# The last output tile taken as three tiles of 128 steps

## The reference

```python
def _moe2_ref(x, w_in, g_ln, w_sg, b_sg, w_out):
    h = gelu_tanh(x @ w_in)                      # (2, 768, 1024)
    u, v = h[..., :512], h[..., 512:]
    v_n = (v - mean(v)) / sqrt(var(v) + 1e-6) * g_ln
    v_s = einsum('ts,bsd->btd', w_sg, v_n) + b_sg[None, :, None]
    gated = u * v_s                              # (2, 768, 512)
    return x + gated @ w_out                     # (2, 768, 384)
```

## Time and profile before

| | before |
|---|---|
| median of 3 executions | 333.68 us (333.19 to 333.71) |
| the profiled execution's own time | 332.61 us |
| its span, first to last instruction | 330.9 us |
| PE busy | 320.0 us, 97% |
| DVE busy | 197.2 us, 60% |
| ACT, POOL busy | 151.0 us, 46%; 98.1 us, 30% |
| mean granted TensorE clock | 0.999 of full speed |
| output transfers L502 | 12 of 192 KB, median 1.9 us from issue to landing |

### The profile page before, as it was taken

The page is one execution under the profiler, slowest core; times in us unless marked ns, Lnnn a source line. Parts: engine busy times, 40 slices in busy tenths (PEclk is TensorE's granted clock), DMA queues, the critical chain, the costliest instruction groups (busy, mean ns, idle before and its releaser), DMA issues.

```text
span 330.9 us, 6786 instructions
## 1 busy us (share of the span) xinstructions
PE 320.0 (97%) x2684; PEld 299.5 (91%) x2684; DVE 197.2 (60%) x331; ACT 151.0 (46%) x301; POOL 98.1 (30%) x94
## 2 busy tenths in 40 slices
PE   6987899999999999999999999999999999999996
PEld 2657889999999999999999998899999988999996
DVE  4869999983696398639416055991643546123432
ACT  5446844553845455465547592755113025311100
POOL 5530344004314211430032050672233018313220
PEclk9999999999999999999999999999999999999999
DMA  7979033232304401300006036000000210000012
GB/s 230 408 259 350 27 124 125 87 130 61 144 2 165 166 5 24 144 9 2 6 9 240 0 110 246 29 0 0 2 0 0 97 49 0 2 0 2 0 48 95
DMA packets 11153, 28.09 MB, mean 85 GB/s; under 512 B 1232, under 2 KB 5872, under 8 KB 9840
## 3 DMA queue, kind: packets, MB, share of 16 engines
q1 hardware_dynamic: 10976, 27.51, 23.7%
q10 hardware_dynamic: 144, 0.14, 0.1%
HBM read 24.74 MB, written 2.36 MB: 82 GB/s over the span
## 4 chain that ended last, share of the span: by engine, by line
PE 84%; DVE 7%; ACT 3%; issue 2%; DMA 2%; POOL 0%; SPq 0%; ACTq 0%; DVEq 0%
PE pm L297 16%; PE pm L298 15%; PE pm L299 15%; PE ps L613 3%; PE ps L297 3%; PE ps L299 3%; PE ps L298 3%; PE py L691 3%; PE pkt L638 3%; PE py L677 2%; PE pkt L297 2%; PE pkt L299 2%; PE pu L297 2%; PE pu L299 2%; PE pkt L298 2%
## 5 line engine op out<-in xcount | busy, mean ns | idle before, releaser
L542 POOL TENSOR_TENSOR k_l<-sq,k_h 128x512 fp32r<-128x512 f32 x24 | 31.9, 1332 | 79.2 <-ACT sq L944 79.2
L297 PE MATMUL pm<-xkr_h,wk_h 128*128 128x256 f32 x144 | 42.1, 292 | 0.0
L297 PE MATMUL pm<-k_h,wv_h 128*128 128x256 f32 x144 | 41.2, 286 | 0.4 <-POOL k_l L542 0.4
L299 PE MATMUL pm<-k_h,wv_l 128*128 128x256 f32 x144 | 40.7, 283 | 0.0
L298 PE MATMUL pm<-k_l,wv_h 128*128 128x256 f32 x144 | 40.7, 283 | 0.0
L298 PE MATMUL pm<-xkr_l,wk_h 128*128 128x256 f32 x144 | 40.7, 283 | 0.0
L299 PE MATMUL pm<-xkr_h,wk_l 128*128 128x256 f32 x144 | 40.7, 282 | 0.0
L533 POOL TENSOR_TENSOR rkp<-inw 128x512 f32<-128x512 f32 x12 | 15.3, 1281 | 62.7 <-DVE r_in L1132 62.7
L936 ACT ACTIVATE relu<-pm 128x512 f32<-128x512 f32 x24 | 14.3, 596 | 36.2 <-PE pm L299 36.1
L595 POOL TENSOR_TENSOR gated_l<-gf,gated_h 128x384 fp32r<-128x384 f32 x16 | 16.4, 1025 | 46.1 <-ACT gated_h L1055 36.1
L1187 DVE SCALAR_TENSOR_TENSOR xf<-X,omu,xf 128x256 f32<-128x256 f32 x36 | 19.5, 554 | 15.4 <-ACT xf L902 15.4
(11 more groups left out here) (239 smaller groups left out, 880.4 us busy)
## 6 DMA issues: line engine op xcount, KB each, us to landing
inw<-in_units SPq DMA_DIRECT2D x10, 1026.5 KB, 5.0
vb<-in_vT SPq DMA_DIRECT2D x12, 256.0 KB, 5.0
wsg_raw<-in_wsgT SPq DMA_DIRECT2D x1, 2304.0 KB, 8.8
out_y<-y_out SPq DMA_DIRECT2D x12, 192.0 KB, 1.9
wk_raw<-in_moe_w_k SPq DMA_DIRECT2D x3, 512.0 KB, 9.9
wv_raw<-in_moe_w_v SPq DMA_DIRECT2D x4, 384.0 KB, 7.0
win_raw<-in_moe_w_in SPq DMA_DIRECT2D x3, 512.0 KB, 4.6
inw<-in_units SPq DMA_DIRECT2D x2, 512.0 KB, 5.5
```

The lines of the kernel that those rows point to most:

```text
L297: pe.matmul(o, a_h, b_h, start=first and n == 0, stop=False, skip_group_check=True)
L299: mm = pe.matmul(o, a_l, b_h, start=False, stop=last and n == len(pairs) - 1, skip_group_check=True)
L542: pool.tensor_tensor(k2_l[:, 2 * n:2 * n + 2], sq[:, j % 2].rearrange("p (g t) -> p g t", g=2), k2_h[:, 2 * n:2 * n + 2], ALU.subtract).th ...
```

## The change

The last entry of the list, ("o", 1, 2, 1), is replaced by three entries ("e", 1, 2, 0), ("e", 1, 2, 1) and ("e", 1, 2, 2). Each covers the same 128 channels and 128 of the 384 steps, and takes the next bank of the ring (7, 0 and 1), one addition of 128 x 128 into the next `y_out` buffer and one transfer of 64 KB. All other tiles keep their order, banks and sizes. The function `out_steps` gives the range of steps of a tile of either kind.

```diff
--- before.py
+++ after.py
@@ -352,6 +352,12 @@
                     ORDER2 += [(x, b, f, h) for h in range(HALVES) for f in range(GT)]
                 if x == "o":
                     ORDER2 += [("o", b, t, h) for h in range(HALVES) for t in range(KT)]
+
+        ORDER2[-1:] = [("e", B - 1, KT - 1, n) for n in range(HALF // C)]
+
+        def out_steps(kind, y):
+
+            return slice(HALF + y * C, HALF + (y + 1) * C) if kind == "e" else slice(y * HALF, (y + 1) * HALF)
         TILES2 = [t for t in ORDER2 if t[0] != "x"]
 
         def filled2(eng, *tile):
@@ -497,10 +503,11 @@
             load_part(sp, len(WSPLIT) - 1)
             n = 0
             for kind, b, x, y in TILES2:
-                if kind == "o":
+                if kind in "oe":
                     emptied2(sp, kind, b, x, y)
-                    sp.dma_start(outT[x * P:(x + 1) * P, b * S + y * HALF:b * S + (y + 1) * HALF],
-                                 y_out[:, n % 3, :]).then_inc(s_out[n % 3], 16)
+                    at = out_steps(kind, y)
+                    sp.dma_start(outT[x * P:(x + 1) * P, b * S + at.start:b * S + at.stop],
+                                 y_out[:, n % 3, 0:at.stop - at.start]).then_inc(s_out[n % 3], 16)
                     n += 1
             for j in range(3):
                 sp.wait_ge(s_out[j], 16 * len(range(j, n, 3)))
@@ -843,8 +850,10 @@
                     if x == 0:
                         pe.wait_ge(gh_done, GT * HALVES * b + GT * (y + 1))
                         pe.wait_ge(gl_done, GT * HALVES * b + GT * (y + 1))
-                    mm = three(pe, o, [((wout_h[:, f, tok], wout_l[:, f, tok]),
-                                        (gated_h[:, f, half], gated_l[:, f, half])) for f in range(GT)], True, True)
+                    at = out_steps(kind, y)
+                    mm = three(pe, o[:, 0:at.stop - at.start], [((wout_h[:, f, tok], wout_l[:, f, tok]),
+                                                                 (gated_h[:, f, at], gated_l[:, f, at]))
+                                                                for f in range(GT)], True, True)
                 mm.then_inc(n_full[bk], 1)
 
         @block.scalar
@@ -1329,11 +1338,13 @@
                         dve.wait_ge(gl_done, ng - 1)
                     dve.tensor_tensor(gf[:, ng % 2], mixed[:, ng % 2], gu[:, x, cols], ALU.mult).then_inc(gf_done, 1)
                     ng += 1
-                elif kind == "o":
+                elif kind in "oe":
+                    at = out_steps(kind, y)
+                    width = at.stop - at.start
                     filled2(dve, kind, b, x, y)
                     if no >= 3:
                         dve.wait_ge(s_out[no % 3], 16 * (no // 3))
-                    dve.tensor_tensor(y_out[:, no % 3], o, x2[:, x, b * S + y * HALF:b * S + (y + 1) * HALF],
+                    dve.tensor_tensor(y_out[:, no % 3, 0:width], o[:, 0:width], x2[:, x, b * S + at.start:b * S + at.stop],
                                       ALU.add).then_inc(n_free[bk], 1)
                     no += 1
```

## The result

| | before | changed |
|---|---|---|
| median of 8 executions each | 333.50 us (333.04 to 333.84) | 334.85 us (333.55 to 335.10) |
| ratio, 95% interval | | 1.0039 (1.0026 to 1.0052) |
| profiled execution, span | 330.9 us | 333.1 us |
| PE busy | 320.0 us, 2684 matmuls | 324.0 us, 2708 matmuls |

One execution of the kernel before, in the series of the first experiments, took 633.67 us; it stands in no comparison here.

A forecast was written before the change was run, and what follows sets the result against it. PE, busy 97% of the span, was taken to bound the kernel. At 0.12 us per narrow matmul the last addition ended +1.90 us, the transfer gave back 0.25, and net +1.65 on 333.68 made 335.3 us, range 333.2 to 336.2.

The forecast's parts named there:

- The 36 loads set PE's time: Last tile on PE: each narrow matmul waits for its weight load, 0.12 us each over 35 steps; 335.3 us, chance 0.65.
- The picture behind it: Weight loads on PE: each begins as the matmul before starts, and the next matmul waits for the whole load, 0.12 us.
- The end of the last matmul: Last narrow matmul on PE: ends 0.23 us after its start against 0.34 before, -0.11 us.
- The addition: Third narrow tile on DVE: 128 columns instead of 384, 0.28 us instead of 0.56, -0.28 us.
- The transfer: Third narrow tile's output: 64 KB instead of 192 KB, -0.25 us taken, range 0 to -0.4.
- The sum: End of the kernel: result of the last addition +1.90 us, transfer gives back 0.25, net +1.65 us.
- The additional code at 0 to 0.1 us: Whole kernel: 24 more matmuls and a handful of waits are more code, with no stall found, 0 to 0.1 us.
- the third addition waits for nothing: Last addition on DVE: its `y_out` buffer, free at about 328.4 us, costs nothing if the third product ends later.
- Load hidden or cheaper: Narrow matmuls on PE: stream sets 0.067 us, or load takes some 0.08; 333.6 to 334.0 us, chance 0.18.
- f32 rate: Narrow matmuls on PE: fp32r below 256 columns runs as f32, 0.213 us each; +4.9 us, 338.6 us, chance 0.13.
- The clock falls: Last two microseconds on PE: clock falls from 2.4 to 1.2 GHz, costing up to 2 us; no chance of its own.

The follow-up runs named there:

- the first experiments: First series of follow-up runs, in which the kernel before was measured too; one of that kernel's executions took 633.67 us.
- the repeated run: The changed kernel measured again with nothing altered: 334.43 us against 333.47 before, ratio 1.0030.
- tail alone: Against the kernel before: the 12 wide matmuls kept, then three additions of 128 columns, each with its 64 KB transfer; 333.20 us, ratio 1.0002.

## Why the prediction was right, point by point

- *The 36 loads set PE's time.* Right, and shown, within what the run with 64 columns of weights leaves open: cadence 0.111 us with 64, 128 and 192 columns, 0.060 with half the weights. The size was taken too high. The nearest row had 0.120 us, but with 192 columns the cadence is 0.111, so at 256 the stream already sets it and that row did not show the load; the f32 loads of 0.11 us, which I had near the low end, had the right number. That is 35 steps by 0.120 = 4.20 us forecast, 3.85 measured, -0.35: 34 steps each 0.0085 us shorter, and the first one 0.06 us instead of 0.12.
- *The picture behind it was too simple.* I wrote that a load begins in the instant in which the matmul before starts, and that a matmul waits for the whole load. In the narrow stream a load begins 0.05 us after a matmul's start (326.71, 326.76) and its own matmul 0.06 us after that. So the 0.12 us between a load and its matmul in rows 6 was no measure of a load either; it is the cadence of 256 columns. What holds is that the loads come one after the other, 0.11 us apart.
- *The end of the last matmul.* 0.28 us after its start, not 0.23. The 0.23 holds where a matmul doesn't wait for its load: 0.22 us for the first narrow one, and for all with 64 columns of weights, where the first addition starts the forecast 0.26 us after its last matmul. In the load-bound stream the record stays at 0.28, and to the addition it is 0.32 instead of 0.26, +0.06.
- *The addition.* 0.29 us for a forecast of 0.28, from a row of the same shape.
- *The transfer.* -0.38 us instead of the -0.25 taken, at the upper end of its bounds (0 to 0.4), as if its length went with the bytes. Median times from issue to landing in the runs: 2.0 us for 256 KB, 1.9 for 192, 1.7 for 128, 1.6 for 96, 1.5 for 64 (1.7 where three were issued close together), 1.4 for 32.
- *The sum.* 1.65 - 0.35 + 0.06 + 0.01 - 0.13 = 1.24 us, the change of L. PE's part cost less and the transfer gave back more than I took, so the time came out below the forecast; the terms themselves were the right ones.
- *The additional code at 0 to 0.1 us.* No time was lost by it in the change, but a late transfer goes with it that I had not seen; it stands in the last section. My statement that the third addition waits for nothing came out true. In the repeated run the second addition did wait for DMA, 0.12 us, off the path.
- *The rivals.* "Load hidden or cheaper" would need a cadence under 0.092. The 0.053 us between the scores' loads fits two loads side by side, 0.107 us for each pair, as the argument against it had it; no run tries that. The price I gave this rival was too low: with a cadence of 0.060 the third addition waited 0.56 us for its buffer, where I had 0.1. Beside these rows, the 81 ns of the Trainium skill's page "TensorE: Matmul & The Clock Gate" (section "Back-to-back issue gap") don't hold for fp32r, where the runs show 111 ns. The same page's section "LDWEIGHTS (loading the stationary operand)" gives the columns of the weights divided by 1.2, in ns; as an estimate by it, 107 for 128 and 53 for 64. The 111 ns of the runs agree with it, and the 60 ns don't contradict it. "f32 rate" is out, by factor two. "The clock falls" had no chance of its own; it is real at 64 columns and absent at 128.

## What to carry to other kernels

A matmul with fresh weights has a floor given by its load, here 0.111 us for 128 columns of fp32r weights at full clock, so cut the moving operand no narrower than the width whose stream covers that floor (of the widths run here 256, with 0.120 us; 192 was at the floor). Price each matmul of a finer last tile by the larger of its load and its stream, not by its columns alone. If a shorter tail is wanted, recut the last two tiles unevenly (512 + 256 for 384 + 384) so that the number of loads stays; here that gave 0.26 us in the traces, less than the medians can show. When a difference is near 0.2%, measure in the trace from the first instruction that differs, since an early dip of the clock moved whole executions of either kernel by about 1 us.

## What the runs showed of the hardware beyond that

**More instructions go with a late transfer.** In the last 8 us of before no instruction transfer runs (q8 has 21 over the whole run), and no output transfer takes more than 2.2 us to land. In every kernel with 12 or more additional matmuls q8 has 22, the last of them among the output transfers, and one of the 192 KB transfers lands 3.2 to 4.2 us after its issue. Before, the change, and the run of the tail alone, which adds no matmul, by their y_out tiles:

```profile
DMA to landing us min/median/max: 1.8/1.9/2.2
```
```profile
DMA to landing us min/median/max: 1.5/1.9/4.0
```
```profile
DMA to landing us min/median/max: 1.6/1.9/2.2
```

The kernels without the additional fetch (before, tail alone, 512 + 256) have no landing above 2.5 us in four traces; the nine traces with it all have one of 3.2 or more. That the one causes the other, by holding one of the 16 engines that share the transfer, is argued from this, not tried. It decides when a buffer comes free: in the run with 64 columns of weights the second narrow addition waited for just such a landing (3.6 us), and the third, until 329.19, for one of ordinary length (issued at 327.06, so 2.1 us). In the change the late landing is hidden under the slow products.

**The load follows the clock.** At a granted clock of 0.50 the load-bound cadence is 0.213 us, against 0.111 at 1.00.
